# The exponentials of two in three query tiles, scaled by the reciprocal row sum on GpSimd in place of VectorE

## The reference

```python
mask = q_bucket[:, :, :, None] == k_bucket[:, :, None, :]   # 6 sign bits of q @ proj and k @ proj
scores = np.where(mask, scale * np.matmul(q, k.transpose(0, 1, 3, 2)), -1000000000.0)
scores = scores - np.max(scores, axis=-1, keepdims=True)
attn = np.exp(scores)
attn = attn / (np.sum(attn, axis=-1, keepdims=True) + 1e-09)
out = np.matmul(attn, v)                    # B=2, H=8, S=768, D=64
x = out.transpose(0, 2, 1, 3).reshape(1536, 512)
x = ((x @ w1) * (x @ w2)) @ w3 @ w_out
y = (1 / (1 + np.exp(-(x @ w_gate))) * (x @ w_val)) @ moe2_w_out
```

## Time and profile before

| | us |
|---|---|
| Median of 3 runs | 819.89 |
| The three runs | 819.89, 815.14, 820.67 |
| Profiled execution: span | 813.6 |
| Attention stage in it, up to the first layer | 0 to about 316 |
| The layers behind | 316 to 813.6 |

### The profile page before, as it was taken

How to read it: one execution, slowest core, us unless ns; L and a number is a source line. 1 busy time by engine, 2 the same in 40 slices (tenths; PEclk the granted TensorE clock), 3 DMA queues, 4 the chain that set the end, 5 groups by cost and what they waited for, 6 DMA issues and landing times.

```text
span 813.6 us, 11907 instructions
## 1 busy us (share of the span) xinstructions
PE 780.8 (96%) x3992; PEld 675.8 (83%) x3992; DVE 385.2 (47%) x888; ACT 381.8 (47%) x678; POOL 232.3 (29%) x146
## 2 busy tenths in 40 slices
PE   6799999999799998999999999999999999999998
PEld 4677887879597887999999888888888888888886
DVE  5799999999999996422222111111111111121220
ACT  5688888888688896323322121222313312221211
POOL 3767365462627332211211121113212312100000
PEclk9999999999999999999999999999999999999999
DMA  6662534537343400100000002002202010000101
GB/s 157 195 168 64 148 84 123 123 94 169 77 113 99 118 28 27 52 27 27 26 0 0 1 27 77 27 2 77 77 1 77 14 63 26 0 26 27 39 26 39
DMA packets 22055, 51.68 MB, mean 64 GB/s; under 512 B 3304, under 2 KB 5992, under 8 KB 22032
## 3 DMA queue, kind: packets, MB, share of 16 engines
q1 hardware_dynamic: 21808, 51.32, 22.5%
q10 hardware_dynamic: 224, 0.07, 0.0%
HBM read 29.43 MB, written 3.15 MB: 40 GB/s over the span
## 4 chain that ended last, share of the span: by engine, by line
PE 80%; DVE 7%; SPq 5%; DMA 5%; issue 2%; ACT 1%; DVEq 0%; ACTq 0%
PE pair_bank L930 14%; PE pair_bank L929 14%; PE pair_bank L928 14%; PE bank L930 6%; PE bank L929 6%; PE bank L928 6%; PE bank L853 5%; PE pair_bank L826 5%; DMA qk_raw<-in_qk 5%; PE bank L838 5%; SPq L218 3%; DVE rowmax L648 2%; DVE pt_lo L681 2%; DVE prob L673 2%; SPq L223 1%
## 5 line engine op out<-in xcount | busy, mean ns | idle before, releaser
L360 POOL TENSOR_TENSOR w_lo<-w_raw,w_hi 128x1024 fp32r<-128x1024 f32 (+1 forms) x36 | 69.5, 1931 | 194.1 <-ACT w_hi L445 192.8
L929 PE MATMUL pair_bank<-x_lo,w_hi 128*128 128x512 f32 (+1 forms) x320 | 117.4, 367 | 0.0
L928 PE MATMUL pair_bank<-x_hi,w_hi 128*128 128x512 f32 (+1 forms) x320 | 117.4, 367 | 0.0
L930 PE MATMUL pair_bank<-x_hi,w_lo 128*128 128x512 f32 (+1 forms) x320 | 117.4, 367 | 0.0
L445 ACT ACTIVATE pt_hi<-bank 128x384 fp32r<-128x384 f32 x192 | 84.9, 489 | 39.3 <-PE bank L838 38.7
L681 DVE TENSOR_TENSOR pt_lo<-bank,pt_hi 128x384 fp32r<-128x384 f32 x192 | 97.6, 549 | 11.7 <-ACT pt_hi L445 11.3
L838 PE MATMUL bank<-ident,prob 128*128 128x128 f32 x576 | 83.5, 280 | 15.8 <-DVE pt_lo L681 14.0
L463 ACT ACTIVATE prob<-pair_bank,ebias,escale 128x768 f32<-128x768 f32 x96 | 95.3, 992 | 5.0 <-DVE ebias L659 5.0
L838 PEld LDWEIGHTS bank<-ident,prob 128*128 128x128 f32 x576 | 67.1, 142 | 35.5 <-DVE pt_lo L681 12.8
L648 DVE TENSOR_REDUCE rowmax<-pair_bank 128x1 f32<-128x768 f32 x96 | 91.2, 950 | 4.3 <-PE pair_bank L826 3.5
L826 PE MATMUL pair_bank<-mk,sq 128*128 128x384 f32 x384 | 89.6, 356 | 1.9 <-ACT prob L463 1.9
(11 more groups left out here) (104 smaller groups left out, 1332.3 us busy)
## 6 DMA issues: line engine op xcount, KB each, us to landing
sq<-hl SPq DMA_DIRECT2D x45, 192.0 KB
w_raw<-in_w SPq DMA_DIRECT2D x32, 256.0 KB, 2.7
mk<-hl SPq DMA_DIRECT2D x15, 384.0 KB
qk_raw<-in_qk SPq DMA_DIRECT2D x7, 768.0 KB, 4.3
wo_raw<-in_wo SPq DMA_DIRECT2D x10, 512.0 KB, 4.1
v_raw<-in_v SPq DMA_DIRECT2D x16, 192.0 KB, 3.4
w_raw<-in_wg SPq DMA_DIRECT2D x12, 256.0 KB, 3.3
w_raw<-in_wv SPq DMA_DIRECT2D x12, 256.0 KB, 3.6
```

What stands on the lines that cost most here:

```text
L360: pool.tensor_tensor(dst, src, hi, ALU.subtract).then_inc(w_ready[j], 1)
L928: pe.matmul(dst, hi, m_hi, start=start, stop=False)
L929: pe.matmul(dst, hi, m_lo, start=False, stop=False)
L930: return pe.matmul(dst, lo, m_hi, start=False, stop=stop)
```

## The change

`normalise` is taken out of VectorE's list and put into GpSimd's as a `tensor_tensor` product with the reciprocal broadcast along the row. Tiles 2, 5, 8 and 11 stay on ScalarE. `qk_split` becomes `qk_hi` and `qk_lo`, and the scalings of tiles 0, 1, 3, 4, 6, 7, 9 and 10 are placed between GpSimd's other tasks; in the looped pairs `w3_split(1, p)` now comes ahead of `attention_sum(p, 0)`. The diff, cut to its core:

```diff
-            def qk_split(p):
+            def qk_hi(p):
...
                 rounded(hl[:, 0::2, :], qk_raw[:, :, :]).then_inc(qk_hi_done, 1)
+
+            def qk_lo(p):
+
                 pool.wait_ge(qk_hi_done, p + 1)
...
+            def normalise(p, *steps):
+
+                for k in steps:
+                    pool.wait_ge(rnorm_done, STEPS * p + k + 1)
+                    pool.tensor_tensor(prob[k % 3][:, :], prob[k % 3][:, :],
+                                       rnorm[:, k:k + 1].broadcast_to([128, SEQ]), ALU.mult).then_inc(norm_done[k % UQ], 1)
+
...
             def pair(p, first=False, last=False):
+                normalise(p, 0, 1)
                 if first:
-                    qk_split(1)
+                    qk_hi(1)
+                    normalise(p, 3)
+                    qk_lo(1)
+                    normalise(p, 4)
                     scale_q_codes(1)
                     w3_split(0, 0, fill_half, 0)
                     wo1_low(0)
+                    normalise(p, 6)
                     wo1_low(1)
+                    normalise(p, 7)
                     v_split(0, 1)
                     w3_split(1, 0, fill_half, 0)
                     wo1_low(2)
+                    normalise(p, 9)
                     wo1_low(3)
+                    normalise(p, 10)
                 else:
+                    w3_split(1, p, wp_done, p)
                     attention_sum(p, 0)
-                    w3_split(1, p, wp_done, p)
+                    normalise(p, 3)
                     if not last:
-                        qk_split(p + 1)
+                        qk_hi(p + 1)
+                    normalise(p, 4)
+                    if not last:
+                        qk_lo(p + 1)
+                    normalise(p, 6)
+                    if not last:
                         scale_q_codes(p + 1)
                     attention_sum(p, 1)
+                    normalise(p, 7)
                     v_split(p, 1)
+                    normalise(p, 9, 10)
                 if not last:
                     w3_split(0, p + 1, fill_half, p + 1)
                     v_split(p + 1, 0)
...
-            def normalise(p, k):
-                dve.wait_ge(rnorm_done, STEPS * p + k + 1)
-                dve.tensor_scalar(prob[k % 3][:, :], prob[k % 3][:, :], rnorm[:, k:k + 1], None,
-                                  ALU.mult).then_inc(norm_done[k % UQ], 1)
-
...
-                    if k % UQ not in NORM_ON_ACT:
-                        normalise(p, k)
```

## The result

| | before | after |
|---|---|---|
| Median, us | 819.93 (4 runs, 815.14 to 820.67) | 828.56 (4 runs, 827.71 to 830.86) |
| Ratio | | 1.0119, 95% interval 1.0081 to 1.0157 |
| Profiled execution: time / span | not given / 813.6 | 828.67 / 826.9 |
| VectorE, GpSimd busy | 385.2, 232.3 | 340.2, 317.8 |

The change makes the kernel slower by 1.2% against this median of before, 8.6 us. The two profiled spans are 13.3 us apart. Both numbers are right: the time of the kernel before varies by itself, as the first experiment explains. What lies around the span is 1.8 us in the profiled execution after (828.67 - 826.9), so the profiled execution of before, at about 815.4 if as much lies around its span, belongs with its fastest.

What follows compares the result with a forecast made beforehand. TensorE sets the pair's length, VectorE close behind, GpSimd seemingly half free. Terms -5.5 + 10.6 + 2.9 + 1.0 = +9.0 us gave span 822.6; the middle of 824.1 and 828.9 gave 826.5 us, range 812 to 836.

Steps and rivals of the forecast that it cites:

- The price: Each scaling product of 128x768 moved to GpSimd costs 1.46 us, like its own q_codes product.
- rival D: Slower: the GpSimd product costs 1.84 us, delaying tiles 3, 4, 6 and 7; 838 us, chance 0.12.
- Tile 4: Looped pair: tile 4's product stands behind tile 3's and qk_hi on GpSimd, so TensorE's transposes stall 0.73 us.
- Tile 7: Looped pair: tile 7's product stands behind tile 6's, scale_q_codes and attention_sum on GpSimd; TensorE stalls 0.84 us.
- SyncE's queue: Looped pair: q_codes comes later, so head 0's DMAs, head 1's issues and the qk_raw load run some 0.2 us late.
- Rival C: Slower: SyncE's queue becomes the bound, 3 us a pair in place of 1.77; 834 us, chance 0.08.
- The first pair: GpSimd's queue is full there; tile 10's transposes come 4 us late, the qk_raw wait takes up 1.1: +2.9 us.
- The last pair: Tile 10's stall goes, but x_lo ends later and the first layer waits, its first products slow: +1.0 us.
- The race: VectorE's tile 3 multiply and GpSimd's hl subtraction exclude each other; removing the multiply saves one lost race, -5.5 us.
- The base: Time around the profiled span of before: about 1.5 or 6.3 us, giving 824.1 or 828.9; the middle was taken.
- Rival B: Stalls at tiles 4 and 7 don't come, as emptier VectorE delivers reciprocals earlier; 812 to 818 us, chance 0.25.

Runs made afterwards that it cites:

- e1: First experiment: kernel before, plus one wait holding GpSimd's subtraction into hl until tile 3's scaling on VectorE is done; 810.05 us, 0.9912 of before.
- e3: Kernel after, with the second attention_sum moved behind the scaling of tile 7 on GpSimd; 833.77 us.
- e4: Kernel after, with SyncE loading the pair after next's qk_raw ahead of head 1's DMAs, in place of behind them; 818.10 us.
- e7: Kernel after, with the early qk_raw load, scale_q_codes ahead of tile 6's scaling and the second attention_sum behind tile 7's; 811.70 us.

## Why the prediction was right, and where its terms were off

**The price** (1.46): measured 1.467. It is the `q_codes` row's price, and it ends rival D's 1.84 and, for this form, the estimate of 1.69 us from the Trainium skill (GPSIMD Engine Reference, Elementwise and Engine selection).

**Tile 4** (0.73): in the pair of 181.4 its transposes start 11.79 us in, where they started 144.52 - 133.48 = 11.04 in: +0.75. **Tile 7** (0.84 more): 20.91 against 19.51, together 1.40 where the sum said 1.57. Both places were right, and the sizes within 0.2 us.

**SyncE's queue** (0.2): head 1's issues at 26.16 against 24.51, +1.65 where the sum said 1.77. So far right. The term that was too small is what comes behind it. From head 1's first issue to that of `qk_raw` it took 6.95 us before and 7.28 now, and from that issue to the sign bits 4.16 and 4.48, with 0.23 us between the two heads' issues where 5.3 lay before. These 0.65 us a pair were in no term: the prediction took the chain behind head 1 as rigid. (That it is slower because head 0's transfers are still under way is argued; no run separates it.) Ordinary pair: 35.6 + 1.77 = 37.4 forecast, 37.8 to 37.9 measured.

**The clock** was in no term for the looped pairs. Behind the wait of 2.25 us at 102.45 TensorE ran at 1.2 GHz; behind that of 2.12 at 181.4 it did not:

```profile
102.40:105.00 2.60, 2.54 (x4) 0.74 (x4) 0.00 (x0) 0.29 (x2) 2.52 (x3) 0.50 0.23 85
181.40:184.00 2.60, 2.60 (x12) 1.60 (x13) 0.83 (x3) 0.36 (x2) 2.52 (x3) 1.00 0.24 87
```

Three of the five complete looped pairs are 0.5 to 1.8 us longer than the ordinary ones, 3.7 in all; two of them (102 and 142) have this clock in them, the third, from 64 us, starts without a wait, has a stall of 1.09 us at tile 4 and ends in the wait of 2.25. The sum: five looped intervals took 193.1 us against 183.9 before, which held 5.5 of lost race, so +14.6 where 5 x 1.77 = 8.9 were forecast. Of the 5.7 too few, 3.7 are these three pairs and 2.0 the ordinary ones. The first and the last pair, below, gave back 1.5, and 13.3 was found where 9.0 was forecast. Rival C (SyncE becomes the bound) was thus half true: its mechanism is at work, as e3 and e4 show, and an ordinary pair pays 2.2 us (37.9 - 35.7) in place of 1.77. It was given too small a chance, and listed as an alternative although the forecast's own sum had already used up SyncE's slack.

**The first pair** (+2.9): +1.9 by the stretches (42.6 against 40.5, 0.2 of it an earlier start). The full queue was there: from tile 3's product at 27.50 to the end of tile 10's at 56.91 GpSimd has no gap. That is 29.4 us where the forecast had 30.4, and this 1.0 us is what the term had too much. The pair of before had also lost time in the race, which the term, counted against that pair, already held; against e1's first pair, 37.7 us, the change costs 4.9.

**The last pair** (+1.0): x_lo was forecast to end 0.4 us behind the old start of the first layer. Counted from the last sign bits the layer starts 70.46 us on, against 69.81, which includes the two tiles' stalls; then its first 24 products take 5.75 in place of 4.17 us, as the first nine or ten of them run at the low clock (0.52 us each in place of 0.33; the granted clock is 0.50 up to 330 us). Together +2.3, where the sixth pair's stalls and the last pair's term made 2.8.

**The race** (-5.5): right, by e1. **The base** was the reason that the median came out well: the forecast, 826.5, took the middle between two readings of what lies around the span. It was 1.8 us, the low reading, by which the forecast would have been 824.4 against 828.56 measured: the sum was 4 us short, and the middle hid half of it. That part was luck. The time also lies just outside what the forecast called no change (811.7 to 828.1, chance 0.48) and within what it called slower (0.40).

**Rival B** (the stalls don't come) fell: VectorE is 4.5 us emptier a pair, and its reciprocals come no earlier: tile 3's starts 5.82 us into the pair in both kernels, tile 6's 15.26 in place of 14.74. It waits instead for ScalarE's high parts, which come behind TensorE's transposes, 52.0 us in all in place of 11.3.

## What to carry to other kernels

Before a step moves to an engine with free time, write down that engine's list with the instant at which each input arrives and each output is wanted; a half-idle engine with a 2.7 us step ahead of a 1.5 us one is late by what the long step leaves. Then follow the outputs that were pushed back, the DMAs behind them too: a stall seen in the profile is worth taking away only if nothing later in the loop takes it over (e3 takes the stall at tile 7 away and loses, e7 takes it away behind an early load and gains). And where executions of one kernel lie in steps apart, look for two instructions that exclude each other; one added wait (e1) gained 0.9%, while the change as it was made lost 1.2%.

## What the runs showed of the hardware

- VectorE's multiply of one SBUF tile by a pointer scalar (610 ns) and GpSimd's work exclude each other, whichever comes first: 3.88 us for the multiply where it starts 0.01 us before a subtraction of 3.46 us, and 3.83 for the subtraction where the multiply came 0.13 us earlier. VectorE's maximum and its subtractions with one operand in PSUM (0.95 and 0.55 us) keep their times beside a busy GpSimd.
- VectorE's sums with both operands in SBUF are hit as well: two of them took 3.75 us beside x_lo in the kernel after (the row at 324.62), one of them 3.28; in the kernel before, with no GpSimd work beside them, they take 0.54 and 0.56 us.
- The Trainium skill (Trainium Architecture — The Big Picture, What this means for kernel authors) calls the port that VectorE and GpSimd share an exclusive lock. The rows above agree, and e1 puts a number on it for a whole kernel: a spread of 11.2 us falls to 2.7.
- The length of an idle time alone didn't tell TensorE's clock behind it. Of the five waits of 2.0 to 2.3 us in the kernel after, three left it at 2.4 GHz (granted clock 1.00) and two sent it to 1.2 for a while (0.50 at 102.4). In e3 it fell behind all five waits of 2.6 to 3.0 us; in the kernel before a wait of 2.99 us at 21.62 left it at 1.00.
